# Loading queries and keys in 32x32 blocks and transposing them on VectorE, in a fused attention and feed-forward kernel

## What is computed

```python
scores = scale * np.matmul(q, k.transpose(0, 1, 3, 2))      # scale = 1/8
rel = pos[:, None] - pos[None, :]
mask_plain = (rel >= 0) & (rel < 32)                          # heads 0 to 3
mask_dil = (rel >= 0) & (rel < 128) & (rel % 4 == 0)          # heads 4 to 7
scores = np.where(masks[None, :, :, :], scores, -1000000000.0)
attn = np.exp(scores - max); attn = attn / (sum + 1e-9)
x = attn @ v                                                  # heads side by side: 512 wide
...
k = np.maximum(xk @ w_k, 0.0)                                 # xk, xr: mixes of a token and the one before
v = k * k @ w_v
x = v / (1.0 + np.exp(-(xr @ w_r)))
...
u = x + (np.maximum(x.T @ w_tok1, 0.0) @ w_tok2).T            # token mixing
out = u + np.maximum(u @ w_ch1, 0.0) @ w_ch2                  # channel mixing
```

## Time and profile before

| | |
|---|---|
| median of 3 runs | 760.42 us (755.93 to 763.25) |
| profiled execution, its own time | 763.75 us |
| its span, first to last instruction | 761.9 us |
| granted TensorE clock, mean | 0.991 of 2.4 GHz |
| busy: PE, DVE, ACT, POOL | 733.7, 365.6, 248.5, 221.5 us |
| attention and first feed-forward block | about 0 to 389 us; the rest has no attention |

### The profile page before, as it was taken

How to read it: one execution, slowest core, us unless ns; L and a number is a source line. 1 busy time by engine, 2 the same in 40 slices (tenths; PEclk the granted TensorE clock), 3 DMA queues, 4 the chain that set the end, 5 groups by cost and what they waited for, 6 DMA issues and landing times.

```text
span 761.9 us, 15692 instructions
## 1 busy us (share of the span) xinstructions
PE 733.7 (96%) x6582; PEld 708.6 (93%) x6582; DVE 365.6 (48%) x624; ACT 248.5 (33%) x623; POOL 221.5 (29%) x237
## 2 busy tenths in 40 slices
PE   7899799999999999999999999999999999999997
PEld 6768799899898989989999999999999999999997
DVE  4486857657476765758673121621326112351222
ACT  3465463543535354353442111311122111231111
POOL 3467664645645464554307200000000000000000
PEclk8899999999999999999999999999999999999999
DMA  9920321221221202020280100110102101010011
GB/s 201 289 50 17 70 61 36 58 54 37 59 60 28 60 19 60 19 63 1 73 321 2 63 16 16 32 63 1 24 10 40 55 1 31 3 32 1 1 32 32
DMA packets 99988, 39.81 MB, mean 52 GB/s; under 512 B 89039, under 2 KB 93519, under 8 KB 99919
## 3 DMA queue, kind: packets, MB, share of 16 engines
q1 hardware_dynamic: 94607, 33.31, 18.6%
q0 software_dynamic: 1088, 4.72, 1.8%
q10 hardware_dynamic: 4224, 0.79, 0.7%
HBM read 29.36 MB, written 4.72 MB: 45 GB/s over the span
## 4 chain that ended last, share of the span: by engine, by line
PE 83%; POOL 6%; issue 3%; DVE 3%; ACT 2%; DMA 1%; ACTq 1%; DVEq 0%; POOLq 0%
PE bank L703 14%; PE bank L704 13%; PE bank L705 13%; PE tq L703 4%; PE tq L705 4%; PE tq L704 4%; PE bank L1140 3%; PE bank L1139 3%; PE s L1140 3%; PE bank L1138 3%; PE s L1138 3%; PE s L1139 3%; PE bank L624 3%; PE bank L588 2%; PE s L498 2%
## 5 line engine op out<-in xcount | busy, mean ns | idle before, releaser
L703 PE MATMUL bank<-xk_hi,WK_hi 128*128 128x288 f32 x224 | 69.5, 310 | 10.7 <-DVE kr L766 8.4
L703 PE MATMUL bank<-k_hi,WV_hi 128*128 128x288 f32 x256 | 78.3, 306 | 0.0
L1115 DVE SCALAR_TENSOR_TENSOR h_lo<-tq,h_hi 128x288 fp32r<-128x288 f32 x48 | 22.0, 458 | 114.1 <-ACT h_hi L1111 114.1
L1115 DVE SCALAR_TENSOR_TENSOR h_lo<-bank,h_hi 128x288 fp32r<-128x288 f32 x48 | 22.0, 457 | 113.4 <-ACT h_hi L1111 113.4
L704 PE MATMUL bank<-k_hi,WV_lo 128*128 128x288 f32 x256 | 75.6, 295 | 0.0
L705 PE MATMUL bank<-k_lo,WV_hi 128*128 128x288 f32 x256 | 75.3, 294 | 0.0
L781 POOL TENSOR_TENSOR k_lo<-kr,k_hi 128x288 fp32r<-128x288 f32 x64 | 53.3, 835 | 71.7 <-ACT k_hi L777 71.4
L704 PE MATMUL bank<-xk_hi,WK_lo 128*128 128x288 f32 x224 | 66.1, 295 | 0.0
L705 PE MATMUL bank<-xk_lo,WK_hi 128*128 128x288 f32 x224 | 65.9, 294 | 0.0
L814 DVE RECIPROCAL rg<-rg 128x288 f32<-128x288 f32 x32 | 62.5, 1953 | 1.1
L1111 ACT ACTIVATE h_hi<-tq 128x288 fp32r<-128x288 f32 x48 | 19.7, 411 | 122.3 <-PE tq L705 122.3
(11 more groups left out here) (163 smaller groups left out, 2112.5 us busy)
## 6 DMA issues: line engine op xcount, KB each, us to landing
C_raw<-in_moe_w_ch SPq DMA_DIRECT2D x6, 1024.0 KB, 11.5
xcur<-X POOLq DMA_DIRECT2D x4, 1152.0 KB, 6.5
out_x<-blocks SPq DMA_DIRECT2D x112, 36.0 KB, 1.7
qraw<-in_q SPq DMA_DIRECT2D x20, 192.0 KB, 3.4
kraw<-in_k SPq DMA_DIRECT2D x20, 192.0 KB, 3.9
vt<-in_v SPq DMA_DIRECT2D x40, 80.0 KB, 2.4
vt<-in_v SPq DMA_DIRECT2D x7, 320.0 KB, 3.3
WK_raw<-in_moe_w_k SPq DMA_DIRECT2D x4, 512.0 KB, 7.8
```

The costliest lines, as they stand in the source:

```text
L703: e.matmul(out_ap, wh, xh, start=start and i == 0, stop=False)
L1115: e.scalar_tensor_tensor(lo, ps, 0.0, hi.bitcast(F32), ALU.max, ALU.subtract).then_inc(Z.h2l_done, 1)
```

## The change

For double chunks 0 to 5 nothing moves. From n = 6 (`NPE`) on:

- Queries and keys are loaded by `load_blocks(n)`: 16 DMAs a double chunk, 24 KB each, in runs of 128 bytes (32 columns of one token), so that a 32x32 block of tokens and columns lies in 32 partitions. It waits until VectorE has read the buffer's former blocks (for n = 6 and 7 until TensorE's transposes of n = 5 are done).
- `transposes(n)` and `evictions(n)` are replaced by `block_transposes(n)`: two VectorE instructions, which transpose the 128x384 blocks of queries and of keys straight into `qT` and `kT`. For odd n their output is strided. They stand in `late[t]`.
- `scores(n)` reads `qT` in another layout, with the same number of matmuls.
- For all n the factor 1/8 leaves the eviction of the queries and becomes the scale of the exponential; the value of masked scores is eight times as large.

```diff
-MASKED = -1.0e9
+MASKED = -8.0e9
+NPE = 6
...
+        def raw_blocks(n):
+
+            return [t[:, DM * (n % 2):DM * (n % 2) + 2 * SU] for t in (qraw, kraw)]
+
+        def load_blocks(n):
+
+            b, j, dil = where(n)
+
+            def sync(e):
+                for src, dst, read, done in zip((q, k), raw_blocks(n), (Z.tq_done, Z.tk_done), (Z.q_done, Z.k_done)):
+                    if n < NPE + 2:
+                        e.wait_ge(read, NPE)
+                    else:
+                        e.wait_ge(done, n - 1)
+                    for s in range(2):
+                        for h in range(2):
+                            for dh in range(2):
+                                r0 = 64 * h + 32 * dh
+                                e.dma_start(dst[r0:r0 + 32, SU * s:SU * (s + 1)].rearrange("p (c d) -> p c d", d=32),
+                                            src[b, 4 * dil + 2 * s + h, SU * j:SU * (j + 1), 32 * dh:32 * dh + 32]
+                                            .rearrange("(c t) d -> t c d", t=32)).then_inc(qk_in[n % 2], 16)
+            return dict(sync=sync)
+
+        def block_transposes(n):
+
+            _, j, dil = where(n)
+            qT, kT = qTs[n % 2], kTs[dil]
+
+            def vector(e):
+                e.wait_ge(qk_in[n % 2], 256 * ((n - NPE) // 2 + 1))
+                wait(e, Z.s_done, n - 1)
+                raws = raw_blocks(n)
+                if dil:
+                    raws = [r.rearrange("p (s i c) -> p s i c", s=2, c=DIL) for r in raws]
+                    dq = qT[:, 0:2 * SU].rearrange("p (s c i) -> p s i c", s=2, c=DIL)
+                    dk = kT[:, :].rearrange("p (s c x) -> p s x c", s=2, c=DIL)[:, :, WINDOW + QB * j:WINDOW + QB * (j + 1), :]
+                else:
+                    raws = [r.rearrange("p (s t) -> p s t", s=2) for r in raws]
+                    dq = qT[:, 0:2 * SU].rearrange("p (s t) -> p s t", s=2)
+                    dk = kT[:, :].rearrange("p (s x) -> p s x", s=2)[:, :, WINDOW + SU * j:WINDOW + SU * (j + 1)]
+                e.transpose(dq, raws[0]).then_inc(Z.q_done, 1)
+                e.transpose(dk, raws[1]).then_inc(Z.k_done, 1)
+            return dict(vector=vector)
...
-                             tq2[:, 0:2 * SU].rearrange("p (g i) -> p g i", g=8), ACT.Copy, scale=0.125).then_inc(Z.q_done, 1)
+                             tq2[:, 0:2 * SU].rearrange("p (g i) -> p g i", g=8), ACT.Copy).then_inc(Z.q_done, 1)
...
+                            q0 = 256 * s + 64 * c if n < NPE else SU * s + QB * c
...
-                                                qT[rows, 256 * s + 64 * c:256 * s + 64 * (c + 1)], keys(rows, s, c),
+                                                qT[rows, q0:q0 + 64], keys(rows, s, c),
...
-                e.activation(sb[:, :], sb[:, :], ACT.Exp).then_inc(Z.e_done, 1)
+                e.activation(sb[:, :], sb[:, :], ACT.Exp, scale=0.125).then_inc(Z.e_done, 1)
...
-            for n in range(4, ND):
-                steps += ([load_v(n)] if n > 4 else []) + ([load_qk(n // 2 + 1)] if n % 2 and n + 1 < ND else [])
+            steps += [load_v(5), load_blocks(6), load_blocks(7)]
+            for n in range(6, ND):
+                steps += [load_v(n)] + ([load_blocks(n + 2)] if n + 2 < ND else [])
...
             for n, t in enumerate(STARTS, 4):
-                late[t].append(transposes(n))
-                early[t + 1].append(evictions(n))
+                if n < NPE:
+                    late[t].append(transposes(n))
+                    early[t + 1].append(evictions(n))
+                else:
+                    late[t].append(block_transposes(n))
                 late[t + 2].append(scores(n))
```

More of the change, by code:

```diff
@@ L162, in build @@
         names = """const_done zeroed mu_in
-            q_in k_in q_in_a q_in_b q_in_1 k_in_a k_in_b k_in_1 v_in0 v_in1 v_in_2 v_in_3 tq_done tk_done q_done k_done s_done masked max_done sub_done e_done sum_done rc_done nm_done
+            q_in k_in q_in_a q_in_b q_in_1 k_in_a k_in_b k_in_1 v_in0 v_in1 v_in_2 v_in_3 qk_in0 qk_in1 tq_done tk_done q_done k_done s_done masked max_done sub_done e_done sum_done rc_done nm_done
             pa_done pb_done pta_done ptb_done o_done x_done
@@ L397, in load_qk @@
             return dict(sync=queries, scalar=keys) if s == 1 else dict(sync=both)
+        qk_in = (Z.qk_in0, Z.qk_in1)
+        def raw_blocks(n):
[34 more added lines that the diff above has]
+            return dict(vector=vector)
         def v_loads(n):
```

## The result

The changed kernel takes 759.6 us (median of 11 runs, 753.34 to 761.6), the kernel before 762.73 us (median of 11). The ratio is 0.9949, 95% interval 0.9927 to 0.9972: half a per cent faster, some 3.9 us, where 5.9 was forecast. The direction and the range were right, the size was not.

What follows compares the result with a forecast made beforehand. TensorE was taken as the bound, with VectorE full in places. Terms +1.9 - 0.67 - 5 x 0.67 - 5 x 0.75 summed to -5.9 us, giving 754.5 us on the runs' scale; 8-in-10 range 747.5 to 762.

Steps and rivals of the forecast that it cites:

- n = 6 and 7: First half batch, where VectorE is full: TensorE's gain worth nothing, two pairs delay its last xk tile, costing 1.9 us.
- What comes to VectorE: Two 384-column transposes per double chunk, 0.47 us each, 0.94 us a pair; bounds from below 0.6 to 2.95 us.
- Unit 5: VectorE only squares there, with idle time between, so TensorE's 0.67 us is gained in full five times.
- wait for L766: TensorE's 1.7 us wait for the squaring, once a half batch in unit 3; no moved instruction in its chain, so it stays.
- a wait for VectorE in units 6 to 8: Sign of being wrong: TensorE waiting for VectorE there would take back the gain at unit 5.
- Units 11 and 18: Five half-batch ends: 0.75 of TensorE's 1.34 us gained each, GpSimd's low parts holding it; new xk_lo wait about 0.6 us.
- the bend: At half-batch ends, beyond pair length p = 1.3 us the last mix itself is late and the end moves by 2p - 2.99.
- the formula: Half batch's end moves by p - 1.69 us up to pair length p = 1.3, and by 2p - 2.99 beyond.
- the loads: SP issues 16 DMAs per double chunk, 0.61 us each, 9.8 us against a 14.8 us period: hidden, costing nothing.
- that rival: Loads late: issues over 0.84 us make SP fall behind; at 0.95 us each, about 772.5 us; chance 0.09.
- TensorE as the bound: Rival: every transpose removed from n = 8 on counts, 10.7 us, 749.7 us, half batches 42.4 us; chance 0.22.
- VectorE held up by GpSimd: Rival: GpSimd blocking or slow strided writes lengthen pairs; 765.5 us at p = 2, 776.8 at 2.95; chance 0.09.

Runs made afterwards that it cites:

- e4: Changed kernel with the block transposes of odd double chunks writing densely instead of strided (results then wrong): ratio 0.9936 to the kernel before.
- e3: Changed kernel with the transpose pair of unit 18 moved one unit later, behind the last mix: ratio 0.9973 to the kernel before.
- e5: Changed kernel with each transpose pair cut to 32 of 384 columns (results then wrong): ratio 0.9871 to the kernel before.
- e6: Changed kernel with two extra VectorE reductions over 128x384 ahead of the pairs at unit 18: ratio 1.0032 to the kernel before.
- e2: Changed kernel with the transpose pair of unit 11 moved two units earlier, into unit 9: ratio 0.9955 to the kernel before.
- e1: Changed kernel with block loads and VectorE transposes only from double chunk 8 on (NPE = 8): 755.18 us, ratio 0.9909 to the kernel before.
- e11: Changed kernel with 8 DMAs of 48 KB in 1536-byte runs per double chunk, not 16 in 128-byte runs (data misplaced): ratio 0.9967 to the kernel before.
- e7: Changed kernel with NPE = 8, pairs moved to units 9 and 19, and later half batches' gate inverses moved: ratio 1.0006 to the kernel before.
- e9: Changed kernel with NPE = 8, unit 11's pair in unit 9, and at unit 18 earlier subtraction and later sums: 752.76 us, ratio 0.9879 to the kernel before.

## Why the prediction was right or wrong

The forecast of -5.9 us against -3.64 at n = 23, term by term:

| term | forecast | measured | with dense output (e4) |
|---|---|---|---|
| n = 6 and 7 | +1.9 | +2.47 | +1.87 |
| n = 8 | -0.67 | -0.64 | -0.61 |
| unit 5, n = 9 | -0.67 | -0.05 | -0.04 |
| unit 5, the other four | -2.68 | -2.50 | -2.51 |
| units 11 and 18, five times | -3.75 | -2.92 | -3.83 |
| sum | -5.9 | -3.64 | -5.12 |

A unit-5 term is the step between the masks of two neighbouring double chunks (8 to 9, 11 to 12, 14 to 15 and so on); the last term is what remains of the step from n = 8 to n = 23. Behind n = 23 the change moves 0.28 us further, for which I have no cause.

**Two steps failed.** The larger is "What comes to VectorE": the price of the pair for odd n. I wrote that the strided output appears in no row, and yet took 0.94 us for all 18 pairs and named "the same length for even and odd n" as the sign of being right. It was 1.34 to 1.45 us for nine of them. That is 1.48 of the 2.26 us that are missing at n = 23 (e4 against the change): 0.60 by n = 7, the rest in the half batches. The price lay inside my bounds (0.6 to 2.95); I should have put the unseen half of the pairs, and not all of them, between the ends.

The smaller is "Unit 5": that TensorE's 0.67 us is gained in full five times. At n = 9 it gave 0.05, because the new wait of 0.38 us for the squaring, 0.65 us by starts, took it back. I had placed the wait for L766 in unit 3, ahead of the start at unit 5, and that holds from the third half batch on. But n = 8 starts at unit 20 and not at 18, so in the second half batch the chain through its sums comes behind the start at unit 5, and the eight transposes had been hiding it. It is the sign of being wrong that I had named, a wait for VectorE in units 6 to 8. With e4 both explain 2.1 of the 2.26 us; the rest is spread over the other terms.

**Units 11 and 18: mechanism right, size off.** GpSimd's low parts hold the end (e3, e5), a new wait of some 0.6 us for `xk_lo` stands there five times (forecast 0.6), and extra work splits by parity as the bend says (e6). With dense pairs each of these steps but the first gave 0.74 or 0.75 us, and the forecast was 0.75. With its own lengths put in, 0.92 and 1.45 us, the formula gives 2.99 - 2.37 = 0.62 us where the odd pair stands at 18, and 1.69 - 1.45 = 0.24 where it stands at 11. Measured are 0.63 and 0.65 at n = 17 and 23, and 0.42 and 0.41 at n = 14 and 20. The second is too low by 0.17 because I took VectorE's two waits as they are written, 0.66 and 0.74 us. By starts they are 0.75 and 0.82 us in the kernel before (168.18 to 169.24 less 0.31 for the product; 171.17 to 173.86 less 1.87 for the inverse), and the odd pair there costs 168.30 - 166.89 = 1.41 us: 1.57 - 1.41 + 0.29 = 0.45. A shorter pair does not give more (e5), since the product with the gate then waits for TensorE, as in e2. At n = 11 the step is 0.81 us, 0.2 more than the formula's 0.62; that is not explained.

**n = 6 and 7.** That TensorE's 1.34 us is worth nothing there and the pairs pass their cost on was right (e1 removes all of it). That 1.9 fits the dense pairs is luck: in e4 the first pair cost 1.84 us by the mask of n = 6 and the second 0.03. The neighbours of the first pair took 0.94 us longer, those of the second 0.72 us less in the change. One of them, the split of weights, has two SBUF inputs, but the gate instruction (L812, L860) has one and still went from 0.26 to 0.66 us here and from 1.38 to 0.77 there. That it is GpSimd that delays them was not tested. That the wait would appear at the last `xk` tile was wrong. TensorE met two longer waits earlier, which put it 91.10 - 88.10 - 0.52 = 2.48 us late, and ran at half clock behind them: at the first `xk` product, 95.71 after and 91.27 before, it was 3.92 us late. That further 1.4 us swallowed the old wait of 1.14 us for `xk_lo`.

**The other four of unit 5, n = 8, the 1.7 us, the loads, ScalarE** went as written: 0.61 to 0.64 us each instead of 0.67; the wait of 1.7 us five times; no wait of VectorE for the blocks of queries or keys, e11 alike. The 16 loads of a double chunk were issued in 7.6 to 10.4 us, 0.47 to 0.65 us each, below the 0.84 us at which SP would have fallen behind. The 0.95 us of that rival was the time of a transfer: here a load landed 2.0 us after its issue while the next was issued after 0.47 us, so transfers overlap and the issue is what counts. The half batches took 43.38 and 43.15 us, where 43.0 was forecast, 44.4 would have been no change and 42.4 TensorE as the bound.

**VectorE held up by GpSimd** did not happen. The even pair took 0.96 us at 179.83 while GpSimd was computing low parts, and 0.92 in the first half batch, and all 36 transposes of e4 lie between 0.519 and 0.570 us. Nor is it GpSimd that makes the odd ones long: in the change the two at 166.89 and 167.58, with GpSimd idle, took 0.83 and 0.86 us. The Trainium skill (SBUF — State Buffer, "Who interferes with whom") lets a VectorE instruction with at most one SBUF input, outside the two-port modes, run without contending with GpSimd. For the block transposes the trace agrees.

## What to carry to other kernels

Moving work from a bounding engine to one that is half idle pays only where the idle time is: the same 0.93 us on VectorE cost 3.9 us in five places at the end of a half batch and 0.5 us elsewhere, and 2.5 us were lost in the one stretch where VectorE was full. Put the moved work where the trace shows idle time, leave out the stretch where there is none (e1), and price each layout that the operation is used with, not only the shape. Before counting removed work as gained, look at the next wait behind it and how much it had to spare: at n = 9 that was 0.22 us, and 0.05 of 0.67 us came. When a wait is taken away by reordering, ask at once what stands behind the thing waited for: here half of 1.7 us came back one engine further on.

## What the hardware showed that I had not expected

- A block transpose of 128x384 with its output columns 192 bytes or more apart takes 0.82 to 0.91 us, densely written 0.52 to 0.57 (e4). By distances that is some 0.72 against 0.47 us. With GpSimd idle the strided ones still took 0.83 and 0.86 us (166.89, 167.58).
- After two waits of 2.71 and 2.48 us with only 5.6 us between their ends, TensorE's granted clock was 0.50 (1.2 GHz of 1.2 and 2.4) for about 2.5 us, and its products started 0.24 us apart instead of 0.13. With waits of 0.83 and 1.86 us in the same places (kernel before), and of 1.51 and 1.85 us (e5), it was not; with 2.71 and 1.90 us (e4) it was. In e7 it was 0.52 on average over 3.5 us behind a wait of 1.58 us.
- The time that the view writes as waiting is less than what is lost: 0.30 us written at n = 17, 0.57 lost by distances; 0.82 written in e9, 1.11 - 0.13 = 0.98 lost.
- With the prologue taken off, the traces of different kernels agree to 0.02 us up to the first instruction that differs (n = 7: 2.47, 2.48, 2.48, 2.49, 2.49, 2.49), while single runs of one kernel differ by over 1%. Effects of half a microsecond were read there and could not have been read from times.
